# Clustered attention and two feed-forward networks: similarity products in two steps of a head, and one-hot work and GpSimd's jobs in other steps

## The reference

```python
q_assign = np.argmax(np.einsum('bhsd,hcd->bhsc', q_n, c_n), axis=-1)
k_assign = np.argmax(np.einsum('bhsd,hcd->bhsc', k_n, c_n), axis=-1)
mask = q_assign[:, :, :, None] == k_assign[:, :, None, :]
scores = np.where(mask, scale * np.matmul(q, k.transpose(0, 1, 3, 2)), -1000000000.0)
attn = np.exp(scores - np.max(scores, axis=-1, keepdims=True))
attn = attn / (np.sum(attn, axis=-1, keepdims=True) + 1e-09)
x = np.matmul(attn, v)                      # 1536 tokens x 512
# first FFN: h = x @ w_in; g = (a0 + a1 h + a2 h^2 + a3 h^3) / (1 + |b0||h| + |b1| h^2 + 1e-6); x = g @ w_out
# second FFN: h = x @ w2_in; x = (h - tanh(h)) @ w2_out
```

## Time and profile before

| | |
|---|---|
| median of 3 runs | 821.57 us (821.53 to 823.38) |
| the profiled execution | 823.63 us, its span 821.8 us |
| TensorE busy | 791.9 us (96%), weight loads 680.3 us |
| VectorE, ScalarE, GpSimd busy | 526.7, 501.5, 353.0 us |
| mean granted TensorE clock | 0.983 of full speed |

### The profile page before, as it was taken

How to read it: one execution, slowest core, us unless ns; L and a number is a source line. 1 busy time by engine, 2 the same in 40 slices (tenths; PEclk the granted TensorE clock), 3 DMA queues, 4 the chain that set the end, 5 groups by cost and what they waited for, 6 DMA issues and landing times.

```text
span 821.8 us, 11654 instructions
## 1 busy us (share of the span) xinstructions
PE 791.9 (96%) x4066; PEld 680.3 (83%) x4066; DVE 526.7 (64%) x910; ACT 501.5 (61%) x954; POOL 353.0 (43%) x377
## 2 busy tenths in 40 slices
PE   5899999999999899999999999999999999999998
PEld 5789998989898787888788888888888888888886
DVE  4599889898988879999977787995311211111111
ACT  3578788888888877878776777777422222222222
POOL 5467787877877723213222222226622222222222
PEclk7699999999999999999999999999999999999999
DMA  4723323332330205200000011115100100001001
GB/s 129 188 72 76 85 73 83 85 77 72 83 74 19 68 11 154 77 0 1 1 0 1 1 51 52 52 52 170 35 1 1 51 1 1 0 9 44 1 0 52
DMA packets 39082, 41.17 MB, mean 50 GB/s; under 512 B 4720, under 2 KB 30320, under 8 KB 39024
## 3 DMA queue, kind: packets, MB, share of 16 engines
q1 hardware_dynamic: 39024, 40.42, 17.5%
HBM read 26.25 MB, written 3.15 MB: 36 GB/s over the span
## 4 chain that ended last, share of the span: by engine, by line
PE 55%; POOL 20%; DVE 13%; issue 6%; ACT 3%; SPq 2%; DMA 1%; POOLq 0%; DVEq 0%; ACTq 0%
PE y_ps L1060 27%; PE h_ps L1039 25%; POOL probs L407 9%; DVE f_bc L841 2%; DVE f_t L860 2%; DVE w_lo L815 2%; DVE f_bc L858 2%; POOL nq L416 2%; DVE f_a L854 2%; POOL v L433 1%; POOL nk L424 1%; POOL hot L441 1%; POOL x_lo L452 1%; DVE f_t L846 1%; POOL hot L442 1%
## 5 line engine op out<-in xcount | busy, mean ns | idle before, releaser
L498 POOL TENSOR_TENSOR g_lo<-f_t,g_hi 128x512 fp32r<-128x512 f32 x96 | 125.1, 1303 | 377.7 <-ACT g_hi L594 377.7
L897 DVE TENSOR_TENSOR f_t<-h_ps,f_a 128x512 f32<-128x512 f32 x48 | 33.2, 691 | 203.4 <-ACT f_a L673 203.4
L1039 PE MATMUL h_ps<-x_hi,w_hi 128*128 128x512 f32 x384 | 149.5, 389 | 1.3 <-DVE w_lo L815 1.3
L1039 PE MATMUL h_ps<-x_lo,w_hi 128*128 128x512 f32 x384 | 149.5, 389 | 0.0
L1039 PE MATMUL h_ps<-x_hi,w_lo 128*128 128x512 f32 x384 | 149.4, 389 | 0.0
L594 ACT ACTIVATE g_hi<-f_t 128x512 fp32r<-128x512 f32 x96 | 60.8, 633 | 138.8 <-PE y_ps L1060 123.4
L407 POOL TENSOR_SCALAR probs<-probs,rinv 128x768 f32<-128x768 f32 x96 | 86.3, 911 | 69.2 <-DVE rinv L782 65.9
L557 ACT ACTIVATE pt_hi<-pt_ps 128x384 fp32r<-128x384 f32 x192 | 85.3, 492 | 48.3 <-PE pt_ps L979 47.1
L788 DVE TENSOR_TENSOR pt_lo<-pt_ps,pt_hi 128x384 fp32r<-128x384 f32 x192 | 98.5, 547 | 13.8 <-ACT pt_hi L557 13.1
L775 DVE TENSOR_REDUCE nmax<-s_ps 128x1 f32<-128x768 f32 x96 | 91.0, 948 | 7.4 <-PE s_ps L966 6.5
L979 PE MATMUL pt_ps<-ident,probs 128*128 128x128 f32 x576 | 85.1, 283 | 6.7 <-POOL probs L407 5.6
(11 more groups left out here) (122 smaller groups left out, 1571.7 us busy)
## 6 DMA issues: line engine op xcount, KB each, us to landing
w_raw<-in_moe_w_in_dram SPq DMA_DIRECT2D x32, 256.0 KB, 2.9
...
```

Source lines behind the costliest of these rows:

```text
L498: pool.tensor_tensor(g_lo[n % 2][:, :], f_t[n % 2][:, :], g_hi[n % 2][:, :].bitcast(F32), ALU.subtract).then_inc(g_lo_done, 1)
L897: dve.tensor_tensor(f_t[n % 2][:, :], h_ps[n % 4][:, :], f_a[n % 2][:, :], ALU.subtract).then_inc(g_done, 1)
L1039: last = pe.matmul(h_ps[n % 4][:, :], w[f][:, ws], x[:, cols], start=(kt == 0 and i == 0), stop=(kt == KT - 1 and i == 2))
```

## The change

Heads 0 to 2 keep their single SIM unit. For heads 3 to 15, SIM becomes SIM_Q (queries, in step 6g - 13, r = 5) and SIM_K (keys, in step 6g - 12, r = 0), six products each, into the two halves of the same area of pr_ps. VectorE reads each half by an instruction of its own (`read_side`): the queries at the end of r = 5, the keys in r = 1 between the two halves of `pt_low`. `read_top` moves from r = 0 to r = 1, and `finish_hot` from r = 3, behind the row maximum, to r = 4, ahead of it. On GpSimd `rank_hot` goes from r = 2 to r = 1, and `split_k` from r = 1 of one head to r = 3, for the head after the next (head 3's stays in step 1). SyncE loads the keys accordingly earlier, head 4's before the weights at the start. The first weight chunk is rounded by ScalarE in step 74, not 78, and split by GpSimd in step 77, not 79.

```diff
-        UNIT_STEP = {HOT: -7, SIM: -13, Q0: -17, Q1: -16, K0: -15, K1: -14}
+        UNIT_STEP = {HOT: -7, SIM: -13, SIM_Q: -13, SIM_K: -12, Q0: -17, Q1: -16, K0: -15, K1: -14}
...
+        def placed(g, u):
+            return (g, u) not in first and not (u == SIM and g > FIRST) and not (u in (SIM_Q, SIM_K) and g <= FIRST)
...
         def wait_copied(engine, g, u):
-            if u == SIM:
-                engine.wait_ge(sim_read, g + 1)
+            if u in SIMS:
+                engine.wait_ge(sim_read, 2 * g + (1 if u == SIM_Q else 2))
...
-        ACT_CHUNK_AT = {78: 0, 80: 1, 84: 2, 88: 3, 94: 4}
-        POOL_CHUNK_AT = {79: 0, 83: 1, 85: 2, 91: 3}
+        ACT_CHUNK_AT = {74: 0, 80: 1, 84: 2, 88: 3, 94: 4}
+        POOL_CHUNK_AT = {77: 0, 83: 1, 85: 2, 91: 3}
...
             load_v(1)
+            sp.wait_ge(k_split, 2)
+            load_k(4)
             sp.dma_start(coef_raw[:, 0:4], poly_a.partition_broadcast(P)).then_inc(coef_in, 16)
...
-                if (k + 15) % T == 0 and 4 <= (k + 15) // T + 1 < HEADS:
-                    g = (k + 15) // T + 1
+                if (k + 27) % T == 0 and 5 <= (k + 27) // T < HEADS:
+                    g = (k + 27) // T
                     sp.wait_ge(k_split, g - 2)
                     load_k(g)
...
-                if r == 1 and 3 <= (k + 17) // T < HEADS:
-                    split_k((k + 17) // T)
-                if r == 2 and 2 <= (k + 10) // T < HEADS:
-                    rank_hot((k + 10) // T)
+                if k == 1:
+                    split_k(FIRST + 1)
+                if r == 1 and 2 <= (k + 11) // T < HEADS:
+                    rank_hot((k + 11) // T)
                 if r == 3 and 1 <= (k + 3) // T < HEADS:
                     split_v((k + 3) // T)
+                if r == 3 and FIRST + 2 <= (k + 21) // T < HEADS:
+                    split_k((k + 21) // T)
...
+            def read_side(g, u):
+                dve.wait_ge(prep_done, prepared(g, u))
+                if u == SIM_Q:
+                    dve.wait_ge(hot_ranked, g - FIRST)
+                side = u - SIM_Q
+                bank = BANK[unit_bank[g, u]]
+                dve.tensor_reduce(sim[:, T * side:T * side + T, :],
+                                  bank[:, side * 2 * T * C:(side + 1) * 2 * T * C].rearrange(
+                                      "p (t j c) -> p t c j", j=2, c=C), AX.X, ALU.add).then_inc(sim_read, 1)
...
                 pt_low(k, 0)
-                if r == 0 and 2 <= (k + 12) // T < HEADS:
-                    read_top((k + 12) // T)
+                if r == 1 and FIRST < (k + 11) // T < HEADS:
+                    read_side((k + 11) // T, SIM_K)
                 pt_low(k, 1)
+                if r == 1 and FIRST <= (k + 11) // T < HEADS:
+                    read_top((k + 11) // T)
+                if r == 4 and 2 <= (k + 8) // T < HEADS:
+                    finish_hot((k + 8) // T)
                 if r == 3 and 2 <= (k + 9) // T < HEADS:
                     read_top2((k + 9) // T)
                 if k + LOOK < TILES:
                     row_max(k + LOOK)
-                if r == 3 and 2 <= (k + 9) // T < HEADS:
-                    finish_hot((k + 9) // T)
                 if k % 2 == 0 and k + 2 < TILES:
                     row_inverse(k + 2, 2)
-                if r == 5 and 2 <= (k + 13) // T < HEADS:
-                    read_sim((k + 13) // T)
+                if r == 5 and FIRST < (k + 13) // T < HEADS:
+                    read_side((k + 13) // T, SIM_Q)
...
-                    for i in range(2 * T):
+                    tiles = {SIM: range(2 * T), SIM_Q: range(T), SIM_K: range(T, 2 * T)}[u]
+                    for i in tiles:
```

More of the change, by code:

```diff
@@ L208, in clustered_attention_then_two_ffns @@
                 "pt0": pt_ps[0][:, :], "pt1": pt_ps[1][:, :], "pv": pv_ps[:, :], "pr": pr_ps[:, :]}
-        Q0, Q1, K0, K1, SIM, HOT = range(6)
+        Q0, Q1, K0, K1, SIM, HOT, SIM_Q, SIM_K = range(8)
         FIRST = 2
@@ L649, in _ @@
                 for g, u in units_at[k]:
-                    if u not in (HOT, SIM):
+                    if u != HOT and u not in SIMS:
                         copy_unit(g, u)
@@ L1069, in _ @@
                 for g, u in units_at[k]:
-                    if u != SIM:
+                    if u not in SIMS:
                         unit(g, u)
```

24 lines of the change are left out of this document (13 added, 11 removed).

## The result

| | before | after |
|---|---|---|
| median of the runs beside each other | 822.29 | 844.58 |
| ratio, 95% interval | | 1.0273 [1.0242, 1.0305] |
| profiled execution / its span | 823.63 / 821.8 | 843.84 / 842.1 |
| steps 6 to 78 | 195.43 | 216.63 |
| a head, mean of twelve | 16.29 | 18.05 |

What follows compares the result with a forecast made beforehand. TensorE was taken as nearly full, the GpSimd chain only a little longer. Twelve heads +5.6, step 6 -0.7, start +0.6, chunk +0.8, step 78 +0.2, clock -0.5 sum to +6.0: 829.6 profiled, 827.6 us median, range 821 to 834.

Steps and rivals of the forecast that it cites:

- (1): In r = 5, six products leave, 3.71 to 3.00 us; r = 0 starts that much earlier; moving finish_hot costs nothing.
- (3): On GpSimd, the 0.56 us wait for the second scaling goes; the stretch taking the key split, 5.0, brings no wait.
- Q0's wait: In r = 1, the next head's unit Q0 waits 1.40 us for VectorE's reading of the key products, in twelve heads.
- r = 5 3.00: Step r = 5 of a head takes 3.00 us, as six similarity products worth 0.71 leave its 3.71.
- r = 0 2.80: Step r = 0 of a head takes 2.80 us: the 2.09 of before and six key products, 0.71.
- r = 1 3.79: Step r = 1 of a head takes 3.79 us, where it was 2.85, because unit Q0 waits.
- the three others: Steps r = 2, 3 and 4 of a head run without waits, at 2.39 us each.
- step 75: Rounding the first weight chunk in step 74 delays ScalarE's pv_part; a 0.36 unit in step 75 fills part: +0.8 us.
- The unit's first load did not run ahead: In r = 1, if Q0's first weight load ran ahead, each wait would be 0.1 us shorter, the time 1.4 less.
- The ends: Outside the twelve heads: step 6 0.7 us earlier, start +0.6, around step 78 +0.2, granted clock 0.5 back.
- A: Rival: in r = 1 Q0's wait is short and the shorter round pays; 810.8 us, faster; chance 0.08.
- C: Rival: each 1.4 us wait in the heads lowers the granted clock, 1.5 each, 18 in all; 845.6 us; chance 0.05.

Runs made afterwards that it cites:

- e3: The kernel after with GpSimd's key split back in r = 1, ahead of the ranking; 833.43 us, ratio to before 1.0134.
- e5: The kernel after with GpSimd's first x_lo of a pair in r = 2, not r = 5; 839.57 us, ratio to before 1.0209.
- e2: The kernel after with VectorE reading the key half ahead of the first low part of r = 1; 831.32 us, ratio to before 1.0106.
- e10: The kernel after with the edits of e2 and e3, and an x_lo behind each of the two scalings of r = 4; 819.63 us.
- e12: e10 with the first weight chunk back in its steps of before, 78 and 79; 818.55 us, ratio to before 0.9943.
- e6: The kernel after with the edits of e2, e3 and e5 together; 820.72 us, ratio to before 0.9965.
- e7: e6 with the first weight chunk back in its steps of before, 78 and 79; 820.28 us, ratio to before 0.9973.
- e8: The kernel before with only the similarity unit split, its two reads, and the maximum read in r = 1; 842.79 us, ratio to before 1.0244.
- e11: e8 with the key half read ahead of the first low part of r = 1; 829.04 us, ratio to before 1.0076.

## Why the prediction was wrong, step by step

**The step that failed** is in (1): "Moving `finish_hot` thus costs nothing, by 0.1". It took `finish_hot` at the 0.78 of the earlier trace rows and carried it to another place. There it takes 1.64, because the key split, which the change puts into r = 3, runs beside it. The same holds of (3), "no wait there": that stretch was weighed for what is queued behind it on GpSimd, not for what runs beside it on VectorE. Measured against e3, 0.88 in r = 5 of eleven of the twelve heads (3.92 and 3.04) and 0.17 in r = 0 of six (2.98 and 2.81): the twelve heads of e3's profile are 10.6 shorter, and its median is 11.1 below after.

**Not in the forecast at all**: `xf` waits for x_lo. With six products and half of a reading less in r = 5, VectorE reaches `xf` sooner, while x_lo still stands behind the scaling of r = 4: 0.88 in six heads, 5.3; e5 measured 5.0. The forecast's terms without these two hold well: 844.6 less e3's 11.1 and e5's 5.0 is an estimate of 828.5 for the change without them, against the 827.6 that was forecast (the two were not taken off together with Q0's wait left in).

**The sum by its own terms**, means of the twelve heads: r = 5 3.00, measured 3.83; r = 0 2.80, measured 3.34; r = 1 3.79, measured 3.60; the three others 7.17, measured 7.27 (0.07 of it is step 75). Forecast 16.76, measured 18.05. The miss of 1.3 a head is 15.5 us, and the twelve heads grew by 21.2 where 5.6 was forecast.

**Right**: Q0's wait, in place, cause and size. It was forecast at 1.40 and is 1.35: the low part began 1.11 after the transposes' load (forecast 1.22), the reading came 0.48 later (0.47) and took 0.35 (0.36), and from Q0's start to the next transposes it was 1.62 (1.67). The unit's first load did not run ahead. e2 confirms the price. Also right: r = 2 to 4 without waits; the half reading, which the Trainium skill, "VectorE: DVE Perf Modes", section "The TRN2 errata", puts at 0.33; and step 75, longer by 0.8 (257.66 to 260.90 is 3.24, against 2.39; it is 3.25 in e10 and 2.41 in e12, which moves the chunks back).

**The ends**: forecast -0.7 + 0.6 ahead of step 6, measured -0.6; behind step 78, forecast 0.2 - 0.5, measured -0.4, and the low clock of the earlier trace rows did not come back (1.00 from 266 to 286). Neither end is confirmed by that. e6 and e7, whose programs are the same up to step 74, reach step 6 at 52.25 and 48.78, so one profile can't tell 0.6 there; and step 78 has the sixth wait of `xf`, 0.9, so that the rest behind it is about 1.3 shorter than before.

**The rivals**: A, a short wait of Q0 and a faster kernel, was ruled out for the order as written, rightly; but it is what one exchanged line gives (e2), and with the holds gone too, the fastest kernel here. C forecast 845.6, the time that came, by another cause: the granted clock of the profiled execution was 0.99, with less than the top digit in only the first two of the page's forty slices, so C is wrong and its number fits by luck. Its price was too high besides: the 1.5 of the earlier trace rows followed on two waits together, and C took 1.5 for each wait.

**What the change is worth** without its side costs: e12, 0.57% below before. Of the +20 of e8, 14 are the order of two lines on VectorE. The other 6 are what is left of two costs, the value split on the first comparison (r = 4 3.31 for 2.28 in e11) and x_lo on `xf` (0.87 in every second head), after what the change gives back in r = 3 and r = 5; no run takes these apart.

**Open**: why 5.5 is missing in the medians of e6 where the heads of the profiles miss 3.7, and whether `nq` could be made in time in e12 (0.3 in six heads); neither was tried.
